# Sparse attention and two feed-forward layers: the order of the three products of a source

## The reference

```python
scores = scale * np.matmul(q, k.transpose(0, 1, 3, 2))
kth = np.partition(scores, -32, axis=-1)[..., -32:-31]
scores = np.where(scores >= kth, scores, -1e9)
attn = softmax(scores); x = attn @ v            # heads side by side: 2304 x 512
h = x @ w_in;  x = np.maximum(0.01 * h, h) @ w_out
h = x @ w2_in
g = np.where(h >= 1, h, np.where(h <= -1, 0.0, (h + 1) ** 2 / 4))
out = g @ w2_out
```

## Time and profile before

| what | us |
|---|---|
| median of 3 timed runs | 1167.02 (1166.76 to 1167.24) |
| span of the profiled execution, first to last instruction | 1165.4 |
| median of the timed runs less that span | 1.6 |
| TensorE busy, products | 1095.4 |
| TensorE busy, weight loads (beside the products) | 1004.5 |
| VectorE busy | 898.2 |
| ScalarE busy | 768.1 |
| GpSimd busy | 465.3 |

### The profile page before, as it was taken

How to read it: one execution, slowest core, us unless ns; L and a number is a source line. 1 busy time by engine, 2 the same in 40 slices (tenths; PEclk the granted TensorE clock), 3 DMA queues, 4 the chain that set the end, 5 groups by cost and what they waited for, 6 DMA issues and landing times.

```text
span 1165.4 us, 21509 instructions
## 1 busy us (share of the span) xinstructions
PE 1095.4 (94%) x7568; PEld 1004.5 (86%) x7568; DVE 898.2 (77%) x2209; ACT 768.1 (66%) x1683; POOL 465.3 (40%) x493
## 2 busy tenths in 40 slices
PE   5558998899999999999999999999999999999998
PEld 3337888799988899899999879988998999999998
DVE  7999999989899998999979989988993005300234
ACT  6886889777678777877768858677875224322332
POOL 4654558552264432643225424124532234222322
PEclk9878999999999999999999999999999999999999
DMA  7997989697656688788667657655455677787763
GB/s 247 346 338 258 396 283 344 217 375 252 237 200 239 233 310 288 279 292 293 232 234 246 227 207 245 211 203 192 160 201 209 209 258 253 256 285 250 257 245 137
DMA packets 90682, 295.53 MB, mean 254 GB/s; under 512 B 10064, under 2 KB 13776, under 8 KB 90576
## 3 DMA queue, kind: packets, MB, share of 16 engines
q1 hardware_dynamic: 86544, 289.45, 70.9%
q10 hardware_dynamic: 4032, 4.72, 1.1%
HBM read 255.85 MB, written 38.27 MB: 252 GB/s over the span
## 4 chain that ended last, share of the span: by engine, by line
PE 64%; DVE 26%; ACT 5%; POOL 2%; issue 2%; DMA 0%; POOLq 0%; SPq 0%; ACTq 0%; DVEq 0%
PE ps_f L927 18%; PE ps_f L935 17%; PE ps_f L928 17%; DVE top L1208 12%; DVE work L1211 10%; PE ps_av L886 5%; PE ps_s L847 2%; DVE part_r L1241 2%; PE ps_t L863 2%; PE ps_t L847 1%; PE ps_t L869 1%; POOL gate L740 1%; POOL part_o L746 1%; ACT probs L1053 1%; ACT probs L1045 1%
## 5 line engine op out<-in xcount | busy, mean ns | idle before, releaser
L1208 DVE MAX8 top<-work 128x8 f32<-128x576 f32 x432 | 310.3, 744 | 0.1
L927 PE MATMUL ps_f<-xy,w_ring 128*128 128x384 f32 (+2 forms) x896 | 290.0, 324 | 5.0 <-DVE bounds L1218 1.6
L935 PE MATMUL ps_f<-gate,w_ring 128*128 128x384 f32 (+2 forms) x896 | 280.8, 313 | 4.9 <-POOL gate L740 4.9
L927 PE MATMUL ps_f<-gate,w_ring 128*128 128x384 f32 (+2 forms) x896 | 285.1, 318 | 0.0
L935 PE MATMUL ps_f<-xy,w_ring 128*128 128x384 f32 (+2 forms) x896 | 281.8, 315 | 2.0 <-POOL xy L750 1.4
L928 PE MATMUL ps_f<-xy,w_ring 128*128 128x384 f32 (+2 forms) x896 | 280.9, 314 | 0.0
L928 PE MATMUL ps_f<-gate,w_ring 128*128 128x384 f32 (+2 forms) x896 | 279.9, 312 | 0.0
L1211 DVE MATCH_REPLACE8 work<-top,work 128x576 f32<-128x576 f32 x288 | 213.4, 741 | 0.0
L740 POOL TENSOR_TENSOR gate<-part_r,gate 128x384 fp32r<-128x384 f32 (+2 forms) x112 | 100.9, 901 | 242.3 <-ACT gate L1112 242.0
L927 PEld LDWEIGHTS ps_f<-xy,w_ring 128*128 128x128 f32 x896 | 170.2, 190 | 19.3 <-issue 9.9
L935 PEld LDWEIGHTS ps_f<-gate,w_ring 128*128 128x128 f32 x896 | 169.2, 189 | 7.1 <-POOL gate L740 7.1
(11 more groups left out here) (86 smaller groups left out, 1845.0 us busy)
## 6 DMA issues: line engine op xcount, KB each, us to landing
w_ring<-w_split SPq DMA_DIRECT2D x408, 512.0 KB, 4.3
w_split<-w_ring SPq DMA_DIRECT2D x40, 512.0 KB, 6.5
raw<-wd SPq DMA_DIRECT2D x64, 256.0 KB, 5.8
w_split<-xy SPq DMA_DIRECT2D x24, 512.0 KB, 4.9
v_sb<-vd SPq DMA_DIRECT2D x32, 320.0 KB, 5.6
kq<-kqd SPq DMA_DIRECT2D x16, 480.0 KB, 4.2
kq<-kqd SPq DMA_DIRECT2D x15, 416.0 KB, 4.6
out_t<-y_acc ACTq DMA_DIRECT2D x12, 192.0 KB, 4.3
```

Of the source, the lines that this page charges most:

```text
L927: pe.matmul(out, w[:, 0, m], high, start=first, stop=False)
L935: mm = pe.matmul(out, w[:, 0, m], low, start=False, stop=end)
L1208: dve.max(top[:, t % T_SLOTS, 8 * r:8 * r + 8], source(t, r)).then_inc(dve_step, 1)
```

## The change

Inside a source block, the second and the third product change places. The wait for the low half of the source stays in front of the first product that reads it, and so moves with it, ahead of the second product. The last product of a unit, which closes the bank and raises `unit_done`, is now the one with the low weights. Nothing else is changed.

```diff
                     pe.matmul(out, w[:, 0, m], high, start=first, stop=False)
-                    pe.matmul(out, w[:, 1, m], high, start=False, stop=False)
                     if opens and u.hidden and not u.layer:
                         pe.wait_ge(x_low_done, gp + 1)
                     elif opens and u.hidden:
                         pe.wait_ge(y_low_done, Y_OF[u.chunk.n, b].y + 1)
                     elif opens:
                         pe.wait_ge(gate_low_done[u.layer], source.in_layer + 1)
-                    mm = pe.matmul(out, w[:, 0, m], low, start=False, stop=end)
+                    pe.matmul(out, w[:, 0, m], low, start=False, stop=False)
+                    mm = pe.matmul(out, w[:, 1, m], high, start=False, stop=end)
```

## The result

The first comparison gave 1169.99 us for the changed kernel (median of 18 runs, 1166.53 to 1172.43) beside 1167.53 us for the kernel before (18 runs, 1165.36 to 1169.33): a ratio of 1.0017, 95% interval 1.0009 to 1.0024, some 2.0 us by the ratio (the medians lie 2.5 us apart). The forecast was 1.1 us, 1168.1 us, and "same". The changed kernel is a little slower, by an amount at the edge of what can be told. The rest of the first comparison's 2.0 us is probably the mix of such falls in its runs; that is not shown, since the clock of those runs of the kernel before is not known.

A forecast was written before the change was run, and what follows sets the result against it. TensorE, mainly its feed-forward products, was taken to bound the kernel. Reordering cost 0, earlier waits 1.5 us, of which 1.1 reach the end: span 1166.5 us, forecast 1168.1 us, range 1164.5 to 1173.5 us.

The forecast's parts named there:

- What bounds the kernel: TensorE holds 64% of the chain of waits, VectorE 26%; feed-forward products 52%, and TensorE is nearly always busy from 900 us.
- three quarters: Share of the 1.5 us of added TensorE time taken to reach the kernel's end, giving 1.1 us.
- The low weights' product in another place: Inside a source, moving this product from second to third place costs 0, its load being hidden beside running products.
- Two neighbours with the same stationary tile: Second and first product of a source now share a tile; taken as 0, since every product has its own load.
- The bounds of 23.8 us less and 197 us more: Extremes for same-tile pairs over 1792 sources: 13.3 ns saved each, or 0.11 us of exposed load each.
- Ten units pay one product each: Opening units with late low halves, 15 waits grouped into 10 units, each lose one 0.150 us step: 1.5 us on TensorE.
- Rival A: In same-tile pairs the second product needs no load of its own; 1152 us, chance 0.13.
- Rival B: Low halves late in nearly all 42 opening units; price 6.3 us, 1173.3 us, chance 0.12.
- The sum: Span 1165.4 + 1.1 = 1166.5 us; runs' median lies 1.6 us above the profiled span, so 1168.1 us.
- Rival C of the prediction: Late products fall into time VectorE or ScalarE sets anyway; median stays at 1167.0 us, chance 0.13.

The follow-up runs named there:

- the pair without the waits: Also "the kernel with the pair only": against the kernel before, new order only in units that do not open a segment, old waits in opening units; 1167.26 us, ratio 1.0006.
- the second comparison: The unaltered change measured again beside the kernel before: 1168.23 us against 1168.72, ratio 1.0005 (0.9996 to 1.0015).
- The ordered growth from none to one to two products: Low-half wait in opening units as before, one or two products earlier: 0, +0.9, +2.3 us at mean clock 0.984; two earlier, old order, 1171.82 us, ratio 1.0031.

## Why the prediction was right

- What bounds the kernel: right. Some 70% of the added products reached the end (1.04 of 1.5 us in the traces, 0.9 to 1.2 us at equal mean clock), where the forecast took three quarters. One reading was wrong and changed nothing: the granted clock is below nine tenths in three of the forty slices (8, 7 and 8), not in one.
- The low weights' product in another place costs nothing: right, shown by the trace of the pair without the waits (no drift against before over 472 sources) and by the unchanged step of 0.1733 us.
- Two neighbours with the same stationary tile cost and save nothing: right, and this was the open point. The bounds of 23.8 us less and 197 us more were wide because no row of before showed such a pair. One row of after settles it: the load at 1154.88 us, one for each product. Rival A fell with it.
- Ten units pay one product each: right. 15 waits before, 15 after, 1.4 us more in them against 1.5; the differences step by 0.11 to 0.19 us right behind them, once for each group of waits. The step of 0.44 us at 689.3 us in the table against before holds both a product and the clock, which fell at 683.3 us there and at 684.8 us in the profile after; against the kernel with the pair only, where it fell at 684.7 us, the step is 0.16 us. The places ahead of 200 us are not checked by this, as the executions compared differ there by steps up and down that are not tied to the waits. Rival B fell: no new wait arose, and the price did not come near 6.3 us.
- The sum: 1.1 us forecast, 1.04 us in the traces, 0.9 to 1.2 us at equal mean clock, 2.0 us in the first comparison and 0.6 us (ratio 1.0005) in the second. The forecast had no term for the falls of the clock that come and go at the openings, 1.6 to 1.7 us each, and its 1168.1 us lies 1.9 us under the measured 1169.99: 0.5 us of it is that the kernel before itself came out at 1167.53 and not 1167.02 us, the rest the larger difference of that comparison. Whether longer waits bring falls more often stays open: the runs' mean clock does not tell which falls a run had.
- Rival C of the prediction, nothing arrives, is refuted by the traces: seven of the eight late places behind 200 us keep their product up to the end. The ordered growth from none to one to two products agrees. Between the medians of the second comparison alone, nothing could be told.

## What to carry to other kernels

Products that share a stationary tile need not stand next to each other: here every product had its load, hidden beside the one before. What the order of products inside a source decides is how much independent work stands ahead of a wait, and each wait that binds pays exactly what is moved behind it. Count late waits by the unit, since waits in a row within a unit paid once here; and if that count matters, add independent work ahead of just those waits, not of all. With effects under 0.3%, subtract the starts of the same instructions in two traces: one product of 0.12 to 0.17 us was plain there, while medians of 11 to 29 runs left it open.

## What the runs showed of the hardware that was not expected

The granted clock falls in the middle of the kernel in some executions and not in others of the same kernel: near 226, 684 and 879 us, each time after a stretch in which TensorE had waited (2.36 us ahead of the first, low gates ahead of the others); it goes to the 1.2 GHz level and comes back. Sixteen value products cost 2.37 or 4.06 us by it, and the kernel before spreads over nearly 5 us (1165.1 to 1169.9 us in 56 runs), to which such falls contribute. The mean clock of a run does not tell them: one of 0.982 had none behind 100 us, one of 0.984 had two. A load of a stationary tile that the product before it had just used is made again, 0.19 us, hidden beside that product, and the next product starts 0.173 us later as always (384 columns).
